# The two MLPs of an attention + MLP + MLP kernel: three rounded fp32r matmuls for each block against one native fp32 product in four 32-column parts, with 512-token tiles

## What is computed

```python
scores = (q @ k.T) / sqrt(64)                       # per batch and head
scores = where(scores >= max(scores) - tau, scores, -1e9)
x = softmax(scores) @ v                             # -> 2304 tokens x 512
h = x @ w_in1;  r = max(h, 0);  x1 = (s * r * r + b) @ w_out1      # 512 -> 2048 -> 512
h = x1 @ w_in2; out = (max(h, 0) + alpha * min(h, 0)) @ w_out2     # 512 -> 2048 -> 512
```

## Time and profile before

| | |
|---|---|
| time, median of 2 runs | 1151.66 us (1150.66 to 1152.66) |
| the profiled execution, its own time | 1150.09 us |
| its span in the profile | 1148.3 us |
| TensorE busy with matmuls | 1118.0 us, 97% of the span |
| attention ends, first MLP begins (first matmul of line 793 in the MLPs) | 336.90 us |
| last matmul begins | 1143.06 us |

### The profile page before, as it was taken

How to read it: one execution, slowest core, us unless ns; L and a number is a source line. 1 busy time by engine, 2 the same in 40 slices (tenths; PEclk the granted TensorE clock), 3 DMA queues, 4 the chain that set the end, 5 groups by cost and what they waited for, 6 DMA issues and landing times.

```text
span 1148.3 us, 20861 instructions
## 1 busy us (share of the span) xinstructions
PE 1118.0 (97%) x6457; PEld 987.4 (86%) x6457; DVE 581.8 (51%) x1159; ACT 534.5 (47%) x1018; POOL 255.1 (22%) x440
## 2 busy tenths in 40 slices
PE   6899999999999999999999999999999999999998
PEld 5666767666669999999999999899999999999997
DVE  6788999999955432423323345532323233232322
ACT  4676777777765432323223245533434333343432
POOL 3454555555557400000000025600000000000000
PEclk9999999999999999999999999999999999999999
DMA  6555556565502200000000004300000000000000
GB/s 155 137 137 133 141 126 148 124 144 129 130 11 74 65 0 0 0 0 0 0 0 0 0 27 128 100 2 1 27 0 27 0 27 0 0 27 0 27 0 27
DMA packets 100110, 59.64 MB, mean 52 GB/s; under 512 B 67040, under 2 KB 83440, under 8 KB 100080
## 3 DMA queue, kind: packets, MB, share of 16 engines
q1 hardware_dynamic: 100080, 59.28, 20.5%
HBM read 30.94 MB, written 4.72 MB: 31 GB/s over the span
## 4 chain that ended last, share of the span: by engine, by line
PE 91%; SPq 4%; issue 2%; DMA 1%; ACT 1%; DVE 1%; ACTq 0%; DVEq 0%
PE psum L793 24%; PE psum L795 24%; PE psum L794 24%; PE psum L899 6%; PE psum L815 4%; PE psum L872 4%; PE psum L817 2%; SPq L349 2%; PE psum L801 1%; PE psum L869 1%; SPq L325 1%; PE psum L880 1%; SPq L328 1%; DMA k_low_half<-k_lo 1%; ACT pt L544 0%
## 5 line engine op out<-in xcount | busy, mean ns | idle before, releaser
L793 PE MATMUL psum<-x_hi,win_hi 128*128 128x384 f32 x768 | 259.4, 338 | 3.0 <-DVE x_raw L757 2.7
L794 PE MATMUL psum<-x_lo,win_hi 128*128 128x384 f32 x768 | 259.0, 337 | 0.0
L795 PE MATMUL psum<-x_hi,win_lo 128*128 128x384 f32 x768 | 259.0, 337 | 0.0
L793 PEld LDWEIGHTS psum<-x_hi,win_hi 128*128 128x128 f32 x768 | 143.9, 187 | 6.9 <-issue 3.0
L794 PEld LDWEIGHTS psum<-x_lo,win_hi 128*128 128x128 f32 x768 | 143.9, 187 | 3.3
L795 PEld LDWEIGHTS psum<-x_hi,win_lo 128*128 128x128 f32 x768 | 143.9, 187 | 0.0
L748 DVE SCALAR_TENSOR_TENSOR act_r<-act_n,nalpha,act_r 128x384 f32<-128x384 f32 x96 | 59.4, 619 | 160.4 <-ACT act_r L599 160.4
L738 DVE SCALAR_TENSOR_TENSOR act_r<-act_r,s_c 128x384 f32<-128x384 f32 x96 | 84.9, 884 | 109.3 <-ACT act_r L590 109.3
L593 ACT ACTIVATE g_hi<-act_r,b_c 128x384 fp32r<-128x384 f32 x96 | 59.2, 617 | 150.3 <-PE psum L795 101.0
L795 PE MATMUL psum<-g_hi,wout_lo 128*128 128x384 f32 x384 | 128.6, 335 | 0.0
L793 PE MATMUL psum<-g_hi,wout_hi 128*128 128x384 f32 x384 | 128.3, 334 | 0.0
(11 more groups left out here) (81 smaller groups left out, 1657.2 us busy)
## 6 DMA issues: line engine op xcount, KB each, us to landing
k_twice<-k_hi SPq DMA_DIRECT2D x64, 144.0 KB, 2.5
stage<-in_moe_w_out_dram SPq DMA_DIRECT2D x32, 256.0 KB, 2.6
k_low_half<-k_lo SPq DMA_DIRECT2D x32, 144.0 KB, 2.4
out_dram<-y_sb SPq DMA_DIRECT2D x18, 256.0 KB, 2.1
raw_q<-in_q_dram SPq DMA_DIRECT2D x32, 128.0 KB, 2.4
raw_k<-in_k_dram SPq DMA_DIRECT2D x32, 128.0 KB, 2.5
raw_v<-in_v_dram SPq DMA_DIRECT2D x32, 128.0 KB, 2.7
q_both<-q_hi SPq DMA_DIRECT2D x32, 128.0 KB, 2.3
```

The lines of the kernel that those rows point to most:

```text
L793: nc.tensor.matmul(dst, lhs[0], rhs[0], start=first, stop=False)
L794: nc.tensor.matmul(dst, lhs[0], rhs[1], start=False, stop=False)
L795: return nc.tensor.matmul(dst, lhs[1], rhs[0], start=False, stop=final)
```

## The change

Attention stays as it is. In both MLPs:

- `three` is replaced by `quarters`: a 128 x 128 block is four `matmul` calls on plain fp32 operands, each with 32 of the 128 weight columns, each writing its own 32 partitions of the same bank. All splits into high and low parts go, on ScalarE, VectorE and GpSimd, and with them `win_hi`, `win_lo`, `wout_hi`, `wout_lo`, `x_hi`, `x_lo`, `g_hi`, `g_lo`.
- A tile has 512 tokens: four full tiles and one of 256 (`REST`). `SKEW` is 3; there are four banks and four slots of `g_sb` for the hidden features.
- `w_in1` and `w_out1` are both loaded during attention, one piece of 256 KB of each for each pair (`load_w1`). `w_in2` and `w_out2` are loaded in eight pieces once attention's output is written, over memory that attention used.
- `square` and the bias step replace `square_relu`; the second layer's leaky step is two VectorE instructions that read PSUM, and ScalarE has only `y_copy` there.
- TensorE's tiles are written out instead of looped.

```diff
-    TOK = 3 * P
-    NT = N // TOK
+    TOK = BANK
+    FULL_TILES = N // TOK
+    REST = N - FULL_TILES * TOK
+    NT = FULL_TILES + 1
+    H_BANKS = 4
+    SKEW = 3
...
-            def load_w_in1(n):
-                sp.dma_start(win_raw[:, :, bass.ts(n, P)], in_chunk(w_in1, n)).then_inc(win_in, DMA)
+            def load_w1(n):
+                sp.dma_start(win1[:, :, bass.ts(n, P)],
+                             w_in1[:, bass.ts(n, P)].rearrange("(c p) f -> p c f", p=P)).then_inc(w1_in, DMA)
+                sp.dma_start(wout1[:, bass.ds(n, 1), :],
+                             w_out1[bass.ts(n, P), :].rearrange("(o p) d -> p o d", o=1)).then_inc(w1_in, DMA)
...
+            sp.wait_ge(o_out, 2 * PAIRS)
+            for c in range(DC):
+                sp.dma_start(win2[:, c, :], w_in2[c * P:(c + 1) * P, :]).then_inc(win2_in, DMA)
+            for c in range(DC):
+                rows = slice(c * FC // DC, (c + 1) * FC // DC)
+                sp.dma_start(wout2[:, rows, :], w_out2.rearrange("(j p) d -> p j d", p=P)[:, rows, :]).then_inc(wout2_in[c], DMA)
...
+            def relu_and_shift(i, j):
+                k, n = i * FC + j, width(i)
+                wait(act, up_done, k + 1)
+                nc.scalar.activation(t_sb[:, j % 2, 0:n], h_bank[j % H_BANKS][:, 0:n], ACT.Relu).then_inc(r_ok, 1)
+                wait_alone(act, down_done, k - H_BANKS + 1)
+                wait(act, t_ok, k + 1)
+                nc.scalar.activation(g_sb[:, j % H_BANKS, 0:n], t_sb[:, j % 2, 0:n], ACT.Identity,
+                                     bias=b_c[:]).then_inc(g_ok, 1)
...
+            def leaky(i, j):
+                k, n = (NT + i) * FC + j, width(i)
+                wait_alone(dve, up_done, k + 1)
+                wait(dve, g_ok, k - 1)
+                h = h_bank[j % H_BANKS][:, 0:n]
+                nc.vector.tensor_scalar(t_sb[:, j % 2, 0:n], h, 0.0, alpha_c[:, j:j + 1], ALU.min,
+                                        ALU.mult).then_inc(t_ok, 1)
+                wait_alone(dve, down_done, k - H_BANKS + 1)
+                wait(dve, t_ok, k + 1)
+                nc.vector.scalar_tensor_tensor(out=g_sb[:, j % H_BANKS, 0:n], in0=h, scalar=0.0, in1=t_sb[:, j % 2, 0:n],
+                                               op0=ALU.max, op1=ALU.add).then_inc(g_ok, 1)
...
+            def quarters(dst, lhs, rhs, first, final):
+
+                for part in (slice(n, n + P // 4) for n in range(0, P, P // 4)):
+                    mm = nc.tensor.matmul(dst[part, :], lhs[:, part], rhs, start=first, stop=final)
+                return mm
+
+            def up(win, layer, i, j):
+                tile = layer * NT + i
+                wait(pe, r_ok if layer == 0 else g_ok, tile * FC + j - H_BANKS + 1)
                 for c in range(DC):
-                    if j == 0:
-                        pe.wait_ge(x_ok, tiles * DC + c + 1)
-                    lhs = [x[:, c, j * P:(j + 1) * P] for x in (win_hi, win_lo)]
-                    rhs = [x[:, c, :] for x in (x_hi, x_lo)]
-                    mm = three(h_bank[j % 2], lhs, rhs, c == 0, c == DC - 1)
+                    mm = quarters(h_bank[j % H_BANKS][:, 0:width(i)], win[:, c, j * P:(j + 1) * P],
+                                x_raw[:, c, tokens(i)], c == 0, c == DC - 1)
                 mm.then_inc(up_done, 1)
...
+                for sub in range(subs(i)):
+                    mm = quarters(acc[sub], g_sb[:, j % H_BANKS, sub * P:(sub + 1) * P], wout2[:, j, :],
+                                j == 0, j == FC - 1)
...
+            pe.wait_ge(w1_in, 2 * PAIRS * DMA)
+            for i in range(NT):
+                layer1_tile(i)
+            pe.wait_ge(win2_in, DC * DMA)
+            for i in range(NT):
+                layer2_tile(i)
```

More of the change, by code:

```diff
@@ L300, in turns_at, with width, tokens, subs @@
                         yield Turn(start.pair, number)
-        def drain_step(n0, l):
-            return l - BODY - UNDER_WAY if static(n0) and n0 == PAIRS - 2 else None
+        def width(i):
+            return REST if static(i) and i == FULL_TILES else TOK
+        def tokens(i):
+            if static(i):
+                return slice(i * TOK, i * TOK + width(i))
+            return bass.ts(i, TOK)
+        def subs(i):
+            return REST_SUB if static(i) and i == FULL_TILES else SUB
         def steps(eng, emit):
@@ L404, in _, with store @@
                 stack(n, n % 2)
-                load_w_in1(n)
+                load_w1(n)
                 load_v(n, n % 2)
[L407 to L422, removed]
+            sp.wait_ge(o_out, 2 * PAIRS)
[4 more added lines that the diff above has]
+                sp.dma_start(wout2[:, rows, :], w_out2.rearrange("(j p) d -> p j d", p=P)[:, rows, :]).then_inc(wout2_in[c], DMA)
+            def store(i):
+                for sub in range(subs(i)):
+                    wait_alone(sp, y_ok[sub], i + 1)
                     sp.dma_start(out[bass.ds(i * TOK + sub * P, P), :], y_sb[:, sub, :]).then_inc(y_out[sub], DMA)
+            with sp.Fori(0, FULL_TILES) as i:
+                store(i)
+            store(FULL_TILES)
             for sub in range(SUB):
-                sp.wait_ge(y_out[sub], DMA * (NT + 1))
+                sp.wait_ge(y_out[sub], DMA * (FULL_TILES + (sub < REST_SUB)))
         @block.gpsimd
@@ L634, in _, with y_copy @@
-            act.wait_ge(acc_free, DC * NT)
-            split_x(0, NT)
-            x1_copy(NT - 1)
-            while m < len(WEIGHTS):
-                split_hi(m)
-                m += 1
-            act.wait_ge(acc_free, DC * (NT + 1))
-            def y_copy(i, last):
+            layer1_tile(0)
+            with act.Fori(1, FULL_TILES) as i:
+                layer1_tile(i)
+            layer1_tile(FULL_TILES)
+            def y_copy(i):
                 wait_alone(act, down_done, FC * (NT + i + 1))
-                for sub in (0, 2):
-                    wait_alone(act, y_out[sub], DMA * (i + 1))
+                for sub in range(0, subs(i), 2):
+                    wait_alone(act, y_out[sub], DMA * i)
@@ L647, in y_copy @@
                     nc.scalar.copy(y_sb[:, sub, :], acc[sub]).then_inc(y_ok[sub], 1)
-            def layer2_tile(i, last):
-                for j in range(FC):
-                    leaky(NT * FC + i * FC + j, j)
-                if not last:
-                    split_x(i + 1, NT + i + 1)
-                y_copy(i, last)
-            with act.Fori(0, NT - 1) as i:
-                layer2_tile(i, False)
-            layer2_tile(NT - 1, True)
+            y_copy(0)
+            with act.Fori(1, FULL_TILES) as i:
+                y_copy(i)
@@ L725, in _, with square @@
             steps(dve, emit)
-            def split_x(src_tile, tiles):
-                for c in range(DC):
-                    wait_alone(dve, x_hi_ok, DC * tiles + c + 1)
-                    nc.vector.tensor_tensor(x_lo[:, c, :], x_raw[:, c, bass.ts(src_tile, TOK)],
-                                            x_hi[:, c, :].bitcast(F32), ALU.subtract).then_inc(x_ok, 1)
-            def square_relu(k, j):
-                r = act_r[:, j % 2, :]
+            dve.wait_ge(const_in, 3 * DMA)
+            def square(i, j):
+                k, n = i * FC + j, width(i)
+                r = t_sb[:, j % 2, 0:n]
                 wait(dve, r_ok, k + 1)
@@ L754, in x1_copy @@
             def x1_copy(i):
                 wait_alone(dve, down_done, FC * (i + 1))
-                for c in range(DC // 2, DC):
-                    nc.vector.tensor_copy(x_raw[:, c, bass.ts(i, TOK)], acc[c][:, 0:TOK]).then_inc(acc_free, 1)
-            split_x(0, 0)
-            dve.wait_ge(o_out, 2 * PAIRS)
-            dve.wait_ge(const_in, 3 * DMA)
-            with dve.Fori(0, NT - 1) as i:
+                for c in range(1, DC, 2):
+                    nc.vector.tensor_copy(x_raw[:, c, tokens(i)], acc[c][:, 0:width(i)]).then_inc(acc_free, 1)
@@ L776, in layer2_tile @@
+            with dve.Fori(1, FULL_TILES) as i:
+                layer1_tile(i)
+            layer1_tile(FULL_TILES)
+            dve.wait_ge(alpha_ok, 1)
+            dve.wait_ge(g_ok, NT * FC)
+            def layer2_tile(i):
                 for j in range(FC):
-                    leaky(NT * FC + i * FC + j, j)
-                if not last:
-                    split_x(i + 1, NT + i + 1)
+                    leaky(i, j)
                 wait_alone(dve, down_done, FC * (NT + i + 1))
-                wait_alone(dve, y_out[1], DMA * (i + 1))
@@ L964, in _, with layer2_tile @@
                     if j >= SKEW:
[L965 to L967 removed]
+                        down1(i, j - SKEW)
+            def layer2_tile(i):
                 for j in range(FC + SKEW):
                     if j < FC:
[L970 removed]
+                        up(win2, 1, i, j)
                     if j >= SKEW:
[L972 removed]
+                        if static(i) and i == 0 and (j - SKEW) % SUB == 0:
+                            pe.wait_ge(wout2_in[(j - SKEW) // SUB], DMA)
+                        down2(i, j - SKEW)
```

236 lines of the change are left out of this document (56 added, 180 removed).

## The result

The changed kernel takes 1332.86 us (1332.52 to 1333.20, 2 runs) against 1151.66: a ratio of 1.157, 95% interval 1.1545 to 1.1601. The forecast was 1337, the range 1320 to 1443. The profiled execution takes 1333.2 us, its span is 1331.4.

The account below looks back on a forecast made before the run. TensorE, busy 97% of the span, was taken as the bound. Attention 336.5 + 1, MLPs 992 and end 4 gave a span of 1333.5 us; with 1.8 and 1.6 us on top, 1337 us, range 1320 to 1443.

Parts of the forecast that it names:

- The block at 1.68 ns a column: MLP matmuls: a native fp32 block costs 0.861 us at 512 columns, 0.430 at 256, 992 us in all.
- Four parts overlap as two do: MLP blocks: four calls of 32 weight columns, eight records, run in two steps, as attention's two heads do.
- The upper bound of 14 ns a step: MLP matmuls: each of 2 x 1248 steps loses 14 ns rather than 2, 30 us more, 1022 us.
- Feeding: Supplying TensorE with 8 matmuls and 8 weight loads a block and its instruction fetches: no cost taken, fetches hidden.
- The bound of 106 us: MLP feeding: if 110 ns is a floor for a pair, short blocks add 86 or 20 us, 106 in all.
- Between `up` and `down`: Relu, square and bias, 2.8 us in all, hide behind 17 us of matmuls; vanished splits gain 3 us, already counted.
- The loads: Attention: `w_out1` issues on SyncE's queue cost 1 us, bounds 0 and 7; `w_in2` and `w_out2` are hidden.
- The end: After the last matmul: one copy and one issue less, 4.0 us in place of 5.0.
- Thin parts faster: MLP matmuls: with 32 weight columns a record takes one column each cycle, kernel 842 us; chance 0.12.
- A floor on pairs: MLP feeding: 110 ns at least per weight load and matmul, kernel 1443 us; chance 0.11, shared with fetches that stick out.
- Two at a time: MLP blocks: only two parts overlap, twice the MLP time, kernel 2329 us; chance 0.03.
- Part of the overlap lost: MLP blocks: third and fourth part add time, a block costs 1.33 times as much, kernel 1667 us; chance 0.03.

Follow-up runs that it names:

- e4_part_outer: The changed kernel with all four chunks of one part in `up` before the next part's: 1847.26 us.
- e3_one_part: The changed kernel with three of a block's four parts left out except in the first call of each sum: 1331.99 us.
- e5_pieces: The changed kernel with the second layer's `up` moving columns cut by tile into pieces of 512, 256, 128, 64 and 256: 1369.57 us.
- e8_native_unrolled: The kernel before with four native fp32 calls a block on the high parts alone and TensorE's tile loops written out: 1336.04 us.
- e2: The changed kernel with each block as one call of all 128 weight columns: 1333.05 us, ratio to before 1.1573.

## Why the prediction was right, by its own steps

- **What bounds it.** Right: TensorE alone. (The three lines of the earlier trace rows add up to 72% and not 71.) Its work grew and the others' shrank, and the time followed TensorE.
- **The block at 1.68 ns a column.** Right: 0.858 us and 0.43 measured against 0.861 and 0.430, and 989 against 992 us for the MLPs. The step that carried the forecast was to read line 899 as records that overlap in two halves, at two cycles a column each. The runs with halves, whole blocks and a single part show the same 0.429 us for each set of records, so the two cycles are the record's own, and neither the width of a part nor the number of parts matters.
- **Four parts overlap as two do.** Taken without a row for it. Right for the order in the change, and by e4_part_outer not in general: this was an assumption that held, not something that the rows of before could show.
- **My reason for it** was that two parts of 64 already fill the array. That was an argument on capacity. e3_one_part shows that it isn't capacity that sets the pace of a part: with three of four parts left out, the rest goes no faster.
- **The upper bound of 14 ns a step** came from fp32r matmuls. It doesn't apply: native records pay 2 to 3 ns with 32, 64 or 128 columns. That bound gave the 1022 us as upper end for the matmuls, where 989 were measured.
- **Feeding.** Right at no cost. The bound of 106 us was far off, for 27 ns a pair is met. Fetches are hidden at the changed kernel's rate, 54 ns a pair and more; they stop being so at about 27 to 29 ns (e5_pieces). A loop with as many calls in its body does stall, 17 us in all, which the prediction did not see. It had the fetches only of written-out code in mind.
- **Between `up` and `down`.** Right: none of it shows. e8_native_unrolled has all the splits and is 3.2 us slower than the changed kernel. Its only waits in the MLPs are 0.45 us at the beginning and 1.39 between the layers, the two places that were counted as gone. An estimate for 1 us of the rest: its 384-token tiles have 2880 steps and the changed kernel 2496, and each step pays 2 to 3 ns.
- **The loads.** 1 us predicted for attention. Its last matmuls start 1.4 us later (334.88, and 333.47 in the earlier trace rows), and the first MLP matmul 1.0 later, as the 0.36 us for `x_lo` is gone. Both are inside the spread; not settled.
- **The end.** 4.0 us predicted, 4.2 measured.
- **Rivals.** Thin parts faster: no (e2, e3). A floor on pairs: no (e5). Two at a time: true only for another order (e4). Part of the overlap lost: no; four records start every 0.429 us, as one does alone, so nothing of the overlap is lost in a long run of parts. The Trainium skill (TensorE: Matmul & The Clock Gate, "Measured speedup vs the span model") has 2.38 times for three column parts, from which the prediction estimated 1.26 times the block's cost; the trace has none of that here.
- **Slips in the working,** none of which moves the forecast. If the third and fourth part each added a third of what a part takes alone, the block would cost 1.67 times as much; 1.33 goes with a sixth each. And 66 ns more on 192 short blocks are 12.7 us, not 12.

## What to carry to other kernels

Count a matmul by distances of starts and by records for each call: a native fp32 call is two records of two cycles a column, so where TensorE is the bound and the splits are hidden, it loses to three fp32r matmuls, here by 23% of the MLPs (989 against 806 us; it would be 33%, four cycles against three, but for the 13 to 14 ns that each fp32r matmul pays on top). Cutting a full 128-column block into parts side by side bought nothing; overlap is of use where columns would stand empty, as with the two heads of attention, and then the parts should follow each other closely in the program. Splits that ran on idle engines cost next to nothing here, so taking them out was no argument for a dearer matmul. If a hardware loop's body grows, look at the packets on the instruction queue and at idle time put down to issue at its turns.

## What the runs showed of the hardware that I had not expected

- Parts of a block overlap four at a time when their calls follow each other, and two at a time when each part has 8 records in a row (1847 us against 1333): the next part starts when the running one has four records left.
- TensorE takes a pair of weight load and matmul every 27 ns for 512 pairs in a row, and at 64 columns one every 14 ns for 128 pairs, then stands for 1.75 us. An instruction packet holds 128 such pairs (44 packets for 5632), and in these stalls one starts 2.3 to 2.9 us before TensorE goes on.
- The turn of a loop over tiles costs 0.99 to 1.84 us when a body has four native calls for each block (8 records), and nothing visible when it has one call, or before's three fp32r matmuls. Packets on the instruction queue: 117 with the stalls, 98 written out, 11 and 13 in the two loops without stalls.
- An fp32r matmul pays 13 to 14 ns beyond its columns, with 128 or 64 weight columns; a native record 2 to 3 ns.
